# A rank matmul, a routing step and a tile layout moved in a three-stage kernel (long convolution, two expert layers) on one Trainium2 core

## The chip, the core and the metric

The kernel runs on one core of one Trainium2 chip. The metric is the device time of one execution in microseconds (us). The core has five engines that run their own instruction streams and meet at semaphores: TensorE (PE in the profile; PEld is its weight load), VectorE (DVE), ScalarE (ACT), GpSimd (POOL) and SyncE (SP), which issues most of the DMAs.

## What is computed

```python
# x, v: (2, 11456, 128); N = 2*11456 = 22912 tokens, D = 128, E = 8 experts, F = 1024
u = x * v;  h_filt = (relu(pos_emb @ w1) @ w2) * exp(-0.01 * pos)
y = causal_convolution(u, h_filt)      # by FFT over the sequence, per channel
x = (x * y).reshape(N, D)
# first expert layer: top-1 of 8
logits = x @ w_gate + modality_bias[modality_id];  e = argmax(logits)
out[t] = softmax(logits)[e] * (relu(x[t] @ w1[e]) @ w2[e])
# second expert layer: the same, routed by cosine similarity to expert_emb over tau
```

## The kernel before, in words

The program has four blocks, one after the other: `attention` (the convolution as small Fourier transforms on TensorE), `first_routing`, `experts` for the first layer (names `moe_...`, `router` true) and `experts` for the second (`moe2_...`). The change touches `first_routing`, `plan_tiles` by its place only, and the TensorE stream of `experts`.

**first_routing** works on `NB` = 184 blocks of 128 rows. TensorE transposes each block (line 951) and multiplies it with the gate weights (line 964), one DMA of 8 blocks at a time (`NU` = 23). The blocks are cut into the groups of `GROUPS`. When all logits of a group are there, VectorE runs `choose(j)` (line 1082 first, one-hot at line 1101), `gates(j)` (line 1108, after ScalarE's exponentials) and `places(j)` (lines 1122 to 1138, after TensorE's two rank matmuls, lines 974 and 975). `due(u)` says after which load TensorE and ScalarE serve a group: three loads after its last block, and never later than the end of the logits. After the last group VectorE works out the place of every row and splits it in a high and a low part, `hi` and `lo`.

Then the **matching loop**, `NM` = 23 rounds of `MG` = 8 blocks. In each, VectorE makes three bfloat16 tiles by comparing and multiplying (`at_lo` line 1188, `at_hi` line 1190, `lo_first` line 1193), ScalarE makes `lo_row` from `at_lo` (line 1036), and TensorE adds 16 matmuls of 208 columns into one bank (lines 992 and 994). The tiles lie in rings of `RING` = 3. Their innermost dimension has `LANES` = 2 blocks interleaved, so that TensorE reads one block with a stride of `LANES` elements. Ahead of the fourth round VectorE runs `plan_tiles`, some 25 small operations (first line 764, last line 808) that work out which tile of 512 rows belongs to which expert; the engines of `experts` read it as loop bounds. The loop ends with a cast of the bank into `k_where` (line 1196).

**experts** runs a loop over tiles of 512 tokens, 47 in the first layer. Per tile TensorE does `up(c)` for c = 0 to 7 (three matmuls each: hidden block c in two-term precision, into `ph`), `down(c)` (three each, accumulated in `po`), `send_back` of the previous tile (line 1440), and in the router layer `send_rank` (lines 697 and 699), which ranks the tokens of the previous tile within their next expert. `down` runs three blocks behind `up`; the third matmul of a `down` waits for VectorE's low part `h_lo` of that block (line 1639; the trace names it with line 1416). ScalarE makes the high part (`h_hi`, line 1518), copies `po` to `oT` (line 1567) when the last down block is done, and then copies `moe_o` to `moe_out` (line 1541, `copy_out`). VectorE fits the router's small operations between its `h_lo`: `factor` (from line 1662, after GpSimd's `moe_norm`, line 1780), `logits`, `best` (one-hot at line 682) and, at the tile's end, `place`. GpSimd takes the root for the norm, gathers the rows of a later tile (line 1761, four DMAs) and, once `moe_out` and the places are there, scatters the previous tile's rows (line 1751, four DMAs). Each engine takes its instructions in the order in which they are written: a wait holds up all that stands behind it.

`send_rank` waits for the one-hot of VectorE and for `moe_o`:

```python
def send_rank(g):
    if router:
        pe.wait_ge(oh_done, g + 1)
        pe.wait_ge(o_done, g + 2)
        r.rank(nc, k, prank).then_inc(rank_done, 1)
```

Of the kernel before, what the change touches and what calls it, by code (L numbers as in the profile page):

```python
# [52 lines left out]
TMAX = (N + NE * (T - 1)) // T  # L53
NHI = TA * (TMAX + 2)
NWG = 104
LANES = 2
ROUND = 1.5 * 2.0 ** 23


# [12 lines left out]
def host_tables():  # L72

    def rows(a, n):
# [27 lines left out]
        "before": f32(np.triu(np.ones((128, 128)), 1)), "not_after": f32(-np.tril(np.ones((128, 128)))),  # L102
        "count": f32(np.tile(np.repeat(np.arange(TA * TMAX), LANES), (128, 1))), "row": f32(np.arange(128) + 1)[:, None],
        "block": f32(128.0 * np.tile(np.arange(NB), (128, 1))), "descend": f32(NE - e), "regions": f32(CAP * e), "origin": f32(CAP * e - (BIG - 1)),
# [715 lines left out]
def first_routing(nc, io, k, att):  # L820
# [3 lines left out]
    XB = 6  # L824
    PB = 3
    GB = 48
    GROUPS = [(0, 48), (48, 48), (96, 48), (144, 32), (176, 8)]
    LATE = 3
    MG = 8
    RING = 3  # L830
    assert NU * UG == NB and sum(n for _, n in GROUPS) == NB
    table = att[1:1 + NB * 128].rearrange("(b p) d -> p b d", p=128)
    with ExitStack() as ctx:
        def sb(name, shape, dt=F32):
            return ctx.enter_context(nc.sbuf_tensor(f"r1_{name}", shape, dt))
# [4 lines left out]
        def sem(name):  # L840
            return ctx.enter_context(nc.semaphore(f"r1_{name}"))
# [24 lines left out]
        oh = sb("oh", [128, NE, NB], BF16)  # L866
        going = {n: sb(f"going{n}", [128, NE, n]) for n in sorted({n for _, n in GROUPS})}
        run = [sb(f"run{j}", [128, NE, n]) for j, (_, n) in enumerate(GROUPS)]
        place = sb("place", [128, NE, GB])
# [6 lines left out]
        lo = sb("lo", [128, NB], BF16)  # L876
        count_f = sb("count_f", [128, TA * TMAX * LANES])
        count = sb("count", [128, TA * TMAX, LANES], BF16)
        row = sb("row", [128, 1])
        first_f = sb("first_f", [128, NB])  # L880
        first = sb("first", [128, NB], BF16)
        at_hi = [sb(f"at_hi{n}", [128, MG // LANES, TA * TMAX, LANES], BF16) for n in range(RING)]
        at_lo = [sb(f"at_lo{n}", [128, MG // LANES, 128, LANES], BF16) for n in range(RING)]
        lo_first = [sb(f"lo_first{n}", [128, MG // LANES, 128, LANES], BF16) for n in range(RING)]
        lo_row = [sb(f"lo_row{n}", [128, MG // LANES, 128, LANES], BF16) for n in range(RING)]
# [27 lines left out]
        counted = sem("counted")  # L913
        planned = sem("planned")
# [3 lines left out]
        def due(u):  # L918

            return [j for j, (b, n) in enumerate(GROUPS) if min((b + n) // UG + LATE, NU + 1) == u]  # L920

# [3 lines left out]
        def _(sp):  # L925
# [8 lines left out]
            sp.dma_start(att[0:1, :], pad[:]).then_inc(meta_out, 16)  # L934
            for j, (b, n) in enumerate(GROUPS):
                sp.wait_ge(gate_done, j + 1)
                sp.dma_start(table[:, b:b + n, D:PITCH], meta[:, b:b + n, :]).then_inc(meta_out, 16)
            sp.wait_ge(meta_out, 16 * (len(GROUPS) + 1))

# [99 lines left out]
        def _(dve):  # L1039
            ch = Chain(dve, chain)  # L1040
# [118 lines left out]
            for e in range(1, NE):  # L1159
# [9 lines left out]
            ch.step(nc.vector.scalar_tensor_tensor(out=lo[:], in0=hi[:], scalar=-128.0, in1=pos[:],  # L1169
                                                   op0=ALU.mult, op1=ALU.add))  # L1170
            ch.settle()
            def lanes(x, m, n):

                return x[:, m * MG:(m + 1) * MG].rearrange("p (c a) -> p c a", a=LANES).unsqueeze(2).to_broadcast(
                    [128, MG // LANES, n, LANES])

            def counts(n):

                return count[:, 0:n, :].unsqueeze(1).to_broadcast([128, MG // LANES, n, LANES])

            for m in range(NM):
                q = m % RING
                if m == RING:
                    plan_tiles(nc, ch, k, counted, planned)
                if m >= RING:
                    dve.wait_ge(matched, m - RING + 1)
                    dve.wait_ge(lo_row_done, m - RING + 1)
                nc.vector.tensor_tensor(out=at_lo[q][:], in0=counts(128), in1=lanes(lo, m, 128), op=ALU.is_equal
                                        ).then_inc(lo_done, 1)
                nc.vector.tensor_tensor(out=at_hi[q][:], in0=counts(TA * TMAX), in1=lanes(hi, m, TA * TMAX),  # L1190
                                        op=ALU.is_equal)
                dve.wait_ge(lo_done, m + 1)
                nc.vector.tensor_tensor(out=lo_first[q][:], in0=at_lo[q][:], in1=lanes(first, m, 128), op=ALU.mult
                                        ).then_inc(hi_done, 1)
# [12 lines left out]
def experts(nc, io, k, name, src, router, dst):  # L1207
# [13 lines left out]
    with ExitStack() as ctx:  # L1221
# [6 lines left out]
        def sem(n):  # L1228
            return ctx.enter_context(nc.semaphore(f"{name}_{n}"))
# [77 lines left out]
        counted = sem("counted")  # L1307
        planned = sem("planned")
# [18 lines left out]
        def total(eng):  # L1327
            return eng.value_load(k.plan[0:1, ENDS + NE:ENDS + NE + 1], min_val=1, max_val=MAXT)
# [65 lines left out]
        @block.tensor  # L1394
        def _(pe):
            pe.sem_inc(xt_done, 1)
            pe.sem_inc(dn_done, HC)
            if router:
                pe.wait_ge(emb_unit, 1)
                nc.tensor.transpose(pback[:, 0, 0:128], emb[:], k.identity[:]).then_inc(emb_turned, 1)  # L1400
                pe.wait_ge(emb_ready, 1)

            def turn(n):

                pe.wait_ge(x_in, n * XN)
                for a in range(TA):
                    mm = nc.tensor.transpose(px[:, a * 128:(a + 1) * 128], x[:, a, 0:D], k.identity[:])  # L1407
                mm.then_inc(xt_done, 1)

            def passes(o, hi, lo, m_hi, m_lo, start, stop, rest):  # L1410

                nc.tensor.matmul(o, hi, m_hi, start=start, stop=False)  # L1412
                nc.tensor.matmul(o, lo, m_hi, start=False, stop=False)  # L1413
                if rest:
                    pe.wait_ge(*rest)
                return nc.tensor.matmul(o, hi, m_lo, start=False, stop=stop)  # L1416

            def up(g, q, c):

                pe.wait_ge(hlo_done, g * HC + (HC + c - 3))  # L1420
                w = slice(c * 128, (c + 1) * 128)
                passes(ph[c % 4][:], w_hi[q][:, 0, w], w_lo[q][:, 0, w], x_hi[:], x_lo[:], True, True,
                       (xlo_done, g + 1) if c == 0 else None).then_inc(up_done, 1)

            def down(g, q, c):
                pe.wait_ge(hhi_done, g * HC + (c + 1))
                w = slice(c * 128, (c + 1) * 128)
                passes(po[:], w_hi[q][:, 1, w], w_lo[q][:, 1, w], h_hi[c][:], h_lo[c][:], c == 0, c == HC - 1,
                       (hlo_done, g * HC + (HC + c + 1))).then_inc(dn_done, 1)

            def send_back(g):

                pe.wait_ge(ot_done, g + 1)
                pe.wait_ge(o_done, g + 1)
                if router:
                    pe.wait_ge(placed, g + 1)
                for a in range(TA):
                    to, cols = pgroups[:, a // 2, a % 2, :], oT[:, a * 128:(a + 1) * 128]
                    if router:
                        mm = nc.tensor.matmul(to, cols, to_rows[:], start=True, stop=True)  # L1440
                    else:
                        mm = nc.tensor.transpose(to, cols, k.identity[:])  # L1442
                mm.then_inc(back_done, 1)
# [7 lines that stand above are left out]
            turn(1)  # L1451

            def body(g, q, s, start):
                pe.wait_ge(w_ready, s * 2 + 1 if router else start * 2 + 1)
                pe.wait_ge(xhi_done, g + 1)
                for c in range(3):
                    up(g, q, c)
                send_back(g)
                pe.wait_ge(w_ready, s * 2 + 2 if router else start * 2 + 2)
                for c in range(3, HC):  # L1460
                    if c == (3 if router else HC - 1):
                        turn(g + 2)
                    up(g, q, c)
                    down(g, q, c - 3)
                down(g, q, HC - 3)
                down(g, q, HC - 2)
                send_rank(g)
                down(g, q, HC - 1)

            sections(pe, None, body)  # L1470
            g = total(pe)
            send_back(g)
            send_rank(g)
# [389 lines left out]
```

## Time and profile before

| | |
|---|---|
| runs | 2071.11, 2071.28, 2074.29 us (median 2071.28) |
| profiled execution | 2071.28 us, of which the span of its instructions 2069.5 us |
| mean granted TensorE clock | 0.961 |
| busy share of the span | TensorE 91%, VectorE 72%, ScalarE 56%, GpSimd 44% |

All times in the rows are microseconds from the start of the span, unless marked ns. A row of the timeline gives start, duration, engine, line, operation, what it writes and reads, shapes, a count where several like ones are merged, and in brackets how long the engine had been idle before it and what released it. The ends of matmuls are modelled, so that one seems to run into the next; the distance of their starts says how fast they come. Matmuls of line 1412, 1413 and 1416 are the first, second and third of an `up` (into `moe_ph`) or a `down` (into `moe_po`).

### The profile page before, as it was taken

The numbers are of one execution on the slowest core, as the hardware profiler recorded it, in microseconds if no ns is written. First come the engines' busy times: TensorE is split into PE (matmuls) and PEld (weight loads), VectorE is DVE, ScalarE is ACT, GpSimd is POOL, SyncE is SP. The second block draws the span as 40 slices with busy tenths as digits, with TensorE's granted clock in tenths as the row PEclk, the third lists the DMA queues.
The fourth block names the chain that finished last, engine by engine and source line by source line (L and its number), as shares of the span: only waits on it lengthen the run. The fifth ranks groups of instructions, "written<-read, shape, count | busy, mean of one in ns | idle before, by whom it ended". The sixth has DMA issues, their size and how long they took to land. (4 is left out here: it accounts for less than half of the span.)

```text
span 2069.5 us, 37272 instructions
## 1 busy us (share of the span) xinstructions
PE 1875.3 (91%) x10049; PEld 1457.8 (70%) x10050; DVE 1482.8 (72%) x3249; ACT 1165.5 (56%) x2462; POOL 909.0 (44%) x879
## 2 busy tenths in 40 slices
PE   8999999999848659999999999984799999999996
PEld 5777777767538547777777777763687787888785
DVE  4759999999925946666666666664677777777775
ACT  1885555555413436666666666553566666666664
POOL 1455555555210036666666666654333232333333
PEclk9999999999969879999999999997899999999998
DMA  2003555555478011111111111124212112111121
GB/s 85 1 24 89 122 123 123 123 123 124 81 168 171 4 61 35 44 44 41 44 44 44 41 45 42 42 59 62 72 46 63 57 46 94 41 46 45 42 64 47
DMA packets 233640, 138.06 MB, mean 67 GB/s; under 512 B 142442, under 2 KB 221364, under 8 KB 233444
## 3 DMA queue, kind: packets, MB, share of 16 engines
q1 hardware_dynamic: 207506, 95.45, 19.9%
q0 software_dynamic: 22080, 39.76, 7.0%
q10 hardware_dynamic: 3986, 2.00, 0.5%
q8 instruction: 37, 0.61, 0.1%
q14 instruction: 31, 0.25, 0.0%
HBM read 96.17 MB, written 43.36 MB: 67 GB/s over the span
## 5 line engine op out<-in xcount | busy, mean ns | idle before, releaser
L1639 DVE SCALAR_TENSOR_TENSOR moe_h_lo<-moe_ph,moe_h_hi 128x512 fp32r<-128x512 f32 x760 | 506.7, 687 | 285.6 <-ACT moe_h_hi L1518 216.2
L1518 ACT ACTIVATE moe_h_hi<-moe_ph 128x512 fp32r<-128x512 f32 x760 | 444.7, 602 | 211.4 <-PE moe_ph L1416 169.9
L1751 POOL DMA_INDIRECT out<-moe_o,moe_idx x200 | 196.9, 984 | 425.5 <-DVE moe_o L1654 361.9
L1412 PE MATMUL moe_ph<-moe_x_hi,moe_w_hi 128*128 128x512 f32 x760 | 320.5, 422 | 18.9 <-issue 16.8
L1416 PE MATMUL moe_po<-moe_h_lo,moe_w_hi 128*128 128x512 f32 x760 | 307.7, 405 | 22.0 <-DVE moe_h_lo L1639 14.6
L1412 PE MATMUL moe_po<-moe_h_hi,moe_w_hi 128*128 128x512 f32 x760 | 304.6, 401 | 0.0
L1416 PE MATMUL moe_ph<-moe_x_lo,moe_w_hi 128*128 128x512 f32 x760 | 302.7, 398 | 0.0
L1413 PE MATMUL moe_ph<-moe_x_hi,moe_w_lo 128*128 128x512 f32 x760 | 301.6, 397 | 0.0
L1413 PE MATMUL moe_po<-moe_h_hi,moe_w_lo 128*128 128x512 f32 x760 | 298.6, 393 | 0.0
L1761 POOL DMA_INDIRECT moe_x<-attention,moe_at x196 | 201.0, 1025 | 208.5 <-issue 195.2
L1751 POOL DMA_INDIRECT rows<-moe_out,moe_r_idx x196 | 195.5, 997 | 181.0 <-ACT moe_out L1541 125.7
L1416 PEld LDWEIGHTS moe_po<-moe_h_lo,moe_w_hi 128*128 128x128 f32 x760 | 143.0, 188 | 87.3 <-DVE moe_h_lo L1639 36.1
L1412 PEld LDWEIGHTS moe_ph<-moe_x_hi,moe_w_hi 128*128 128x128 f32 x760 | 145.0, 191 | 59.5 <-issue 35.6
L320 PEld LDWEIGHTS ps<-dft_rows_sb,W 107*119 107x119 f32 x1536 | 172.4, 186 | 19.9 <-issue 19.9
L320 PE MATMUL ps<-dft_rows_sb,W 107*119 107x108 f32 x1536 | 177.7, 270 | 6.7 <-DVE W L450 5.5
L1416 PEld LDWEIGHTS moe_ph<-moe_x_lo,moe_w_hi 128*128 128x128 f32 x760 | 144.6, 190 | 34.6 <-DVE moe_x_lo L1625 0.2
L1413 PEld LDWEIGHTS moe_po<-moe_h_hi,moe_w_lo 128*128 128x128 f32 x760 | 143.2, 188 | 31.4
L1567 ACT ACTIVATE moe_oT<-moe_po 128x512 f32<-128x512 f32 x95 | 56.8, 598 | 192.1 <-PE moe_po L1416 192.1
L1413 PEld LDWEIGHTS moe_ph<-moe_x_hi,moe_w_lo 128*128 128x128 f32 x760 | 145.3, 191 | 25.2
L1412 PEld LDWEIGHTS moe_po<-moe_h_hi,moe_w_hi 128*128 128x128 f32 x760 | 143.2, 188 | 28.1 <-ACT moe_h_hi L1518 0.3
L333 PE MATMUL ps<-A,dft_cols_sb 119*109 119x432 f32 x384 | 155.3, 526 | 0.3 <-DVE POOLED L482 0.3
L590 POOL TENSOR_TENSOR U<-X,V 107x440 f32<-107x440 f32 x64 | 71.8, 1122 | 176.7 <-DVE POOLED L527 174.3
(210 smaller groups left out, 3165.5 us busy)
## 6 DMA issues: line engine op xcount, KB each, us to landing
moe_x<-rows SPq DMA_DIRECT2D x49, 260.0 KB
X<-in_x SPq DMA_DIRECT2D x64, 192.5 KB, 5.3
V<-in_v SPq DMA_DIRECT2D x64, 192.5 KB, 4.2
XF<-in_xf SPq DMA_DIRECT2D x64, 192.5 KB, 2.6
moe_w_raw<-in_moe_w SPq DMA_DIRECT2D x24, 512.0 KB
r_x<-attention SPq DMA_DIRECT2D x23, 512.0 KB, 6.8
attention<-POOLED SPq DMA_DIRECT2D x48, 220.0 KB
out<-moe_o,moe_idx POOLq DMA_INDIRECT x200
```

Of the source, the lines that this page charges most:

```text
L320: mm = nc.tensor.matmul(p[0:KW, a, c * 2 * H1:(c + 1) * 2 * H1], W[g % 2][0:N1, a, c, 0:KW], dft_rows[0:N1, :], start=True, stop=True)
L333: mm = nc.tensor.matmul(p[0:N2, x, 0:F4], dft_cols[0:KW, x * N2:(x + 1) * N2], A[g % 2][0:KW, :, :, x, :].rearrange("p a c f -> p (a c) f" ...
L590: nc.gpsimd.tensor_tensor(out=U[t % 2][:, 0], in0=X[t % NX][0:N1], in1=V[t % NX][0:N1], op=ALU.mult).then_inc(u_ready, 1)
L1412: nc.tensor.matmul(o, hi, m_hi, start=start, stop=False)
L1413: nc.tensor.matmul(o, lo, m_hi, start=False, stop=False)
L1416: return nc.tensor.matmul(o, hi, m_lo, start=False, stop=stop)
L1518: nc.scalar.activation(h_hi[c][:], ph[c % 4][:], ACT.Relu).then_inc(hhi_done, 1)
L1567: nc.scalar.activation(oT[:], po[:], ACT.Copy).then_inc(ot_done, 1)
L1639: nc.vector.scalar_tensor_tensor(out=h_lo[c][:], in0=ph[c % 4][:], scalar=0.0, in1=h_hi[c][:].bitcast(F32), op0=ALU.max, op1=ALU.subtract) ...
L1751: pool.indirect_dma_start(dst, bass.IndirectOffsetOnAxis(ap=idx[:, a:a + 1].bitcast(U32), axis=0), out[:, a, 0:width], None, bounds_check= ...
L1761: pool.indirect_dma_start(x[:, a, :], None, src, bass.IndirectOffsetOnAxis(ap=at[:, a:a + 1].bitcast(U32), axis=0), bounds_check=NB * 128, ...
```

## The change

Four edits. `LANES` goes from 2 to 4: the tiles of the matching loop interleave four blocks instead of two, and the table `count` (and the input it is cast from) doubles. `GROUPS` has a last group of 40 blocks in place of one of 32 and one of 8. `plan_tiles` is called ahead of the matching loop instead of ahead of its fourth round. In `experts`, `send_rank(g)` is called ahead of the last three down blocks instead of ahead of the last one.

```diff
-LANES = 2
+LANES = 4
...
-    GROUPS = [(0, 48), (48, 48), (96, 48), (144, 32), (176, 8)]
+    GROUPS = [(0, 48), (48, 48), (96, 48), (144, 40)]
...
             ch.settle()
+            plan_tiles(nc, ch, k, counted, planned)
+
             def lanes(x, m, n):
...
             for m in range(NM):
                 q = m % RING
-                if m == RING:
-                    plan_tiles(nc, ch, k, counted, planned)
                 if m >= RING:
...
                     up(g, q, c)
                     down(g, q, c - 3)
+                send_rank(g)
                 down(g, q, HC - 3)
                 down(g, q, HC - 2)
-                send_rank(g)
                 down(g, q, HC - 1)
```

## Rows read from the trace of the kernel before

**Rows 1.** The page, busy us (share of the span) and instructions, TensorE
```profile
PE 1875.3 (91%) x10049; PEld 1457.8 (70%) x10050; DVE 1482.8 (72%) x3249; ACT 1165.5 (56%) x2462; POOL 909.0 (44%) x879
```

**Rows 2.** Windows: busy us and count by engine, clock, DMA share, GB/s
```profile
664.23:679.64 15.41, 0.68 (x4) 0.24 (x4) 13.96 (x51) 0.67 (x2) 0.00 (x0) 0.66 0.47 72
679.64:735.10 55.46, 41.02 (x368) 35.22 (x368) 53.30 (x92) 26.44 (x23) 0.00 (x0) 0.91 0.00 1
```

**Rows 3.** Timeline of the groups, first operation of each and the last logits
```profile
619.33 0.56 DVE L1082 TENSOR_TENSOR r_lg<-r_psl,r_bias 128x384 f32<-128x384 f32 x1 [5.08 <-PE r_psl L964]
...
660.50 3.72 PE L964 MATMUL r_psl<-r_wg,r_xT 128*128 128x104 f32 x32
...
664.23 0.42 DVE L1082 TENSOR_TENSOR r_lg<-r_psl,r_bias 128x256 f32<-128x256 f32 x1
...
670.57 0.22 DVE L1082 TENSOR_TENSOR r_lg<-r_psl,r_bias 128x64 f32<-128x64 f32 x1
...
674.17 0.16 DVE L1148 TENSOR_SCALAR r_room<-r_run 128x8 f32<-128x8 f32 x1
```

**Rows 4.** Timeline of VectorE: plan_tiles and the start of two rounds
```profile
686.06 0.15 DVE L764 TENSOR_TENSOR k_nth<-k_cursor,k_origin 1x8 f32<-1x8 f32 x1
...
690.08 0.69 DVE L1188 TENSOR_TENSOR r_at_lo<-r_count,r_lo 128x1024 bf16<-128x1024 bf16 x1
...
692.23 0.68 DVE L1188 TENSOR_TENSOR r_at_lo<-r_count,r_lo 128x1024 bf16<-128x1024 bf16 x1
```

**Rows 5.** Matching loop, groups by form (busy us, mean ns, idle before); two matmuls
```profile
L1190 DVE TENSOR_TENSOR r_at_hi<-r_count,r_hi 128x1664 bf16<-128x1664 bf16 x23 | 23.4, 1018 | 0.0
L994 PEld LDWEIGHTS r_psx<-r_at_hi,r_lo_row 128*128 128x128 bf16 x184 | 19.0, 103 | 0.6
...
L1188 DVE TENSOR_TENSOR r_at_lo<-r_count,r_lo 128x1024 bf16<-128x1024 bf16 x23 | 15.8, 685 | 0.0
...
724.85 0.25 PE L992 MATMUL r_psx<-r_at_hi,r_lo_first 128*128 128x208 bf16 x1
...
724.94 0.25 PE L994 MATMUL r_psx<-r_at_hi,r_lo_row 128*128 128x208 bf16 x1
```

**Rows 6.** Timeline, router layer: one h_lo, TensorE's down blocks 5 and 7, the rank
```profile
1009.10 0.68 DVE L1639 SCALAR_TENSOR_TENSOR moe_h_lo<-moe_ph,moe_h_hi 128x512 fp32r<-128x512 f32 x1
...
1009.84 0.50 PE L1416 MATMUL moe_po<-moe_h_lo,moe_w_hi 128*128 128x512 f32 x1 [0.18 <-DVE moe_h_lo L1639]
...
1011.52 0.19 PE L697 MATMUL moe_pback<-moe_r_oh,k_before 128*128 128x40 bf16 x1
...
1011.66 0.48 PE L1412 MATMUL moe_po<-moe_h_hi,moe_w_hi 128*128 128x512 f32 x1
...
1011.97 0.40 PE L1413 MATMUL moe_po<-moe_h_hi,moe_w_lo 128*128 128x512 f32 x1
...
1012.21 0.40 PE L1416 MATMUL moe_po<-moe_h_lo,moe_w_hi 128*128 128x512 f32 x1
```

**Rows 7.** The same tile and the next one-hot, other engines
```profile
1007.18 0.17 DVE L1662 TENSOR_SCALAR moe_scale<-moe_norm 128x4 f32<-128x4 f32 x1 [1.60 <-POOL moe_norm L1780]
...
1010.33 0.19 DVE L682 TENSOR_TENSOR moe_r_oh<-k_descend,moe_r_km 128x32 bf16<-128x32 f32 x1
...
1011.36 1.01 POOL L1761 DMA_INDIRECT moe_x<-attention,moe_at  x1 [0.30 <-issue]
...
1013.13 0.63 ACT L1541 ACTIVATE moe_out<-moe_o 128x520 f32<-128x520 f32 x1
...
1023.75 0.19 DVE L682 TENSOR_TENSOR moe_r_oh<-k_descend,moe_r_km 128x32 bf16<-128x32 f32 x1
```

**Rows 8.** Timeline of ScalarE at the end of the next tile
```profile
1026.61 0.60 ACT L1567 ACTIVATE moe_oT<-moe_po 128x512 f32<-128x512 f32 x1 [2.75 <-PE moe_po L1416]
1027.10 0.64 ACT L1541 ACTIVATE moe_out<-moe_o 128x520 f32<-128x520 f32 x1
```

**Rows 9.** Groups of ScalarE, 780 to 1360 us; idle before in us
```profile
L1567 ACT ACTIVATE moe_oT<-moe_po 128x512 f32<-128x512 f32 x42 | 25.1, 598 | 104.6 <-PE moe_po L1416 104.6
```

## The prediction

> **What bounds the kernel now.** I read the page first [rows 1]: TensorE is busy 91% of the span, so most of the kernel is TensorE work that this change leaves alone. Its granted clock dips in one place, between the attention and the first expert layer, and three of the four edits are there. So I took windows by stage [rows 2]: from 664.23 to 679.64 us, where the routing numbers are made, TensorE works 0.68 us and VectorE 13.96 of 15.41; from 679.64 to 735.10, the matching loop, VectorE works 53.30 of 55.46 us and TensorE 41.02. VectorE is the bound of both. The fourth edit is in the first expert layer, which I read tile by tile in the timeline [rows 6, 7].
>
> In such a tile TensorE's third matmul of down block 5 waits 0.18 us at 1009.84 for VectorE's h_lo. VectorE is late because it had waited 1.60 us for GpSimd's norm (row at 1007.18). GpSimd is late because it first issues four scatters of the tile before, and these wait for ScalarE's copy to moe_out. That copy waits for oT, and oT for TensorE's last down matmul. So there is a closed loop: one-hot (its end, called T here, is 1010.33 + 0.19 = 1010.52), last down matmul 1012.21, copy 1013.13, scatters, norm, one-hot again at T = 1023.94. That is 13.42 us a tile, and TensorE's small stalls are its slack. Whatever lies between T and the copy counts in full, once a tile.
>
> **The parts.**
>
> *Five groups become four, the last of 40.* Groups 0 to 2 keep their sizes. Now VectorE takes the group of 32 from 664.23 to 670.57, 6.34 us, and the group of 8 to 674.17, 3.60, together 9.94 [rows 3]. Both are the same chain of small operations, so the cost per block is (6.34 - 3.60) / 24 = 0.114 us, and 40 blocks take 6.34 + 8 x 0.114 = 7.25. What is lost is a head start: the new group needs the very last logits, whose matmuls end at 660.50 + 3.72 = 664.22. VectorE comes free at 664.23 anyway, so with a handover it starts at 664.3. Gain 9.94 - 7.25 - 0.09 = **2.6 us**; the ends are 2.2 (a later handover, or one return from another engine that is late) and 2.8.
>
> *plan_tiles ahead of the loop.* It is 4.0 us of VectorE (686.06 to 690.08) wherever it stands [rows 4]. VectorE runs the 23 rounds of 2.15 us (690.08 to 692.23) almost without a wait, so the sum is the same. TensorE now starts 4 us later, with the same work per round, and the final matmuls follow VectorE's last round as before. **0**, from -0.2 (TensorE no longer pauses in mid-loop) to +0.5 (its first rounds, at the half clock, use up the ring of three).
>
> *LANES 2 to 4.* The same instructions over the same elements; only the order inside a tile changes, and the stride at which TensorE reads, from 4 to 8 bytes. VectorE takes 1018 ns for the 1664 elements of at_hi and 685 for the 1024 of at_lo [rows 5]: 640 more in 333 ns, 1.92 per ns. If a pair per step is its full rate, runs of four bring nothing; I expect no gain. TensorE's matmuls come 0.09 us apart (724.85, 724.94) and may take 2.15 / 16 = 0.134 before they set the pace. No row has an 8-byte stride. The lower end is 0.09, no cost. For the upper I take the widest reads in the trace: 512 contiguous four-byte columns every 0.235 us [rows 6] are 8.7 bytes of range per ns, and 208 columns at 4 bytes in 0.09 are 9.2. If range were the limit, 8 bytes would take 0.19, a round 3.04, and 21 rounds 21 x 0.89 = 19 us more. I take the lower end, because per column both rows are alike too (2.2 and 2.3 per ns), that is, skipping every second element has cost nothing so far. The weight loads (103 ns) lie beside the matmuls. The table of counts doubles, 0.2 MB more; its load and cast lie in VectorE's idle time before 619.33, 5.08 us [rows 3]. **0**.
>
> The Trainium skill, page "SBUF — State Buffer", section "Door 1: The DMA port swizzle", says that SBUF is read in lines of 16 bytes and that the full rate needs at least two hits in a line. Eight bytes are just at that limit: by the rule the edit costs 0 and the sum stands, by the upper bound it would be 19 us more. No row here shows it.
>
> *The rank moved ahead of two down blocks.* It takes its wait for the one-hot along, and what stands behind it in TensorE's queue, down blocks 5, 6 and 7 and then the next tile, waits too. Down 4 is issued by about 1009, one-hot comes at 1010.52: TensorE stands still for 1.5 us (about 1.0 once the period has grown). Before, it did blocks 5 and 6 in that time. New timing from T, by the gaps of [rows 6]: start of the rank +0.06 (h_lo ends 1009.78, its matmul starts 1009.84), first down matmul +0.14, second +0.31, third +0.24, six more at 0.235 = 1.41. The last starts at T + 2.16, where it was T + 1.69. So **+0.47 us on the loop** for a tile like this.
>
> But there are two kinds of tile. In this one the copy starts at 1013.13, T + 2.61. In the next [rows 8] it starts at 1027.10, T + 3.16, with the down matmuls no later after T: their release comes late. ScalarE's mean idle before oT over 42 tiles is 104.6 / 42 = 2.49 us [rows 9]; between 2.20 for the prompt kind (1012.64 less the end of its x_hi copy at 1010.44) and about 2.75 for the late one, that makes some 20 prompt tiles and 22 late. oT starts there at 1026.61, T + 2.67. GpSimd's fourth gather starts 1011.36, T + 0.84 in every tile I looked at, so I read the late release as tied to GpSimd's work, about 1.8 us after that gather began, and not to the matmul. Then the late tiles lose nothing: the new last matmul ends at 2.16 + 0.40 = T + 2.56, still before it. They may gain up to 0.1. Sum: 21 prompt tiles (one more near the end of the layer) x 0.47 = 9.9, less 22 x 0.05 = 1.1 for the late, **+8.8 us**. Ends: 7.7, and 43 x 0.47 = 20.2 if the lateness adds to the matmul.
>
> *Sum.* 2071.28 (the profiled run's own time, which is also the median of the three; its span is 2069.5) - 2.6 + 0 + 0 + 8.8 = **2077.5**.
>
> **Rivals.** *The lateness adds to the matmul:* I don't see what holds the release back, and if it is something of TensorE's own it will still come after the last matmul. Against it: its time fits GpSimd's. 2071.3 - 2.6 + 20.2 = 2088.9.
>
> *The moved rank costs nothing.* A TensorE that pauses may post its releases at once in every tile, and this would pay the 9.9 back: 22 late tiles x 0.55 = 12.1, less the 1.1 already counted, offsets most or all of it. Or the pace of the layer is held elsewhere. 2071.3 - 2.6 = 2068.7.
>
> *TensorE becomes the bound of the matching loop,* by the 8-byte stride and above 0.134 us a matmul. 2077.5 + 19 = 2096.5. For it: no row reads so wide a range; against: columns, not range, have set the pace so far.
>
> *Faster:* the rank's increment, queued ahead of down 7's, is what holds the release; moved away it clears all 22 late tiles, 12.1 us, and the wait is hidden as well. It decides only if the one-hot is there when down 4 ends, 1.5 us earlier after the norm than the rows show. 2071.3 - 2.6 - 12.1 = 2056.6.
>
> **How the numbers follow.** The forecast has 0.50, with a range of its own of 2075 to 2081; lateness adds 0.17; the rank costs nothing 0.13; stride 0.10; faster 0.08; the last 0.02 is what I can't name. A measurement of this kernel can tell about 0.2% from no change, 4.1 us. Slower by more: 0.50 + 0.17 + 0.10 = 0.77; within: 0.13 + 0.02 = 0.15; faster: 0.08. The range leaves out the stride and the faster case: 2068 to 2090, holding 0.80.
>
> **What would show it.** In the new profile the rank's first matmul, line 697, waits for VectorE's one-hot in nearly every tile, about 1 us each; every copy to moe_out starts T + 3.05 to 3.2, and the period is 13.9 us in all tiles; VectorE does the last group from 664.3 to about 671.6; a round of the loop stays 2.14 to 2.15 us with matmuls 0.09 apart, and VectorE's last round ends 2.6 us earlier. What would make it wrong: copies at T + 3.6 (lateness adds), rounds near 3 us (stride), no wait ahead of line 697, or copies at T + 2.6 in all tiles.

## The result, and the profile after

| | before | after |
|---|---|---|
| median (lowest to highest), us | 2072.78 (2071.11 to 2074.86), 4 runs | 2103.27 (2100.5 to 2107.57), 4 runs |
| ratio, 95% interval | | 1.0148 (1.0128 to 1.0170) |
| profiled execution, its span | 2071.28, 2069.5 | 2087.48, 2085.7 |

Slower by 1.5%, 30.5 us, where the forecast was 2077.5 and the range ended at 2090. The profiled execution of the changed kernel lies 16 us below its timed runs. The runs below came on three chips, here A (the first four kernels), B (the next four) and C (the last four), on which the kernel before took 2045.52 (15 runs), 2075.59 (15) and 2048.17 (29). What differs between them is in the first expert layer and behind it, and the profile of the changed kernel looks there like chips A and C, that of before like chip B. So this profile is compared with that of before ahead of that layer, and from there on with care.

The page of the changed kernel, the line of busy times, beside [rows 1]:

```profile
PE 1883.0 (90%) x10047; PEld 1469.6 (70%) x10048; DVE 1480.7 (71%) x3231; ACT 1169.9 (56%) x2461; POOL 908.9 (44%) x879
```

Almost nothing is to be seen there, since it is an average over stages. The same two stages as in [rows 2], as windows of the changed kernel (columns as there), show it:

```profile
665.23:681.96 16.73, 0.45 (x2) 0.11 (x2) 15.32 (x56) 0.47 (x1) 0.00 (x0) 0.62 0.43 66
681.96:753.52 71.56, 69.23 (x368) 43.25 (x368) 50.91 (x71) 26.44 (x23) 0.00 (x0) 0.95 0.00 1
```

The matching loop holds fewer VectorE instructions than before, 71 for 92, since plan_tiles has left it, and yet takes 71.56 us where it took 55.46. TensorE works 69.23 us of it for 41.02, with the same 368 matmuls: the bound has changed engines. The timeline of VectorE from the last group to the first round answers to [rows 3, 4]:

```profile
665.23 0.49 DVE L1082 TENSOR_TENSOR r_lg<-r_psl,r_bias 128x320 f32<-128x320 f32 x1
...
672.48 0.16 DVE L1148 TENSOR_SCALAR r_room<-r_run 128x8 f32<-128x8 f32 x1
...
677.94 0.15 DVE L764 TENSOR_TENSOR k_nth<-k_cursor,k_origin 1x8 f32<-1x8 f32 x1
...
681.96 0.68 DVE L1188 TENSOR_TENSOR r_at_lo<-r_count,r_lo 128x1024 bf16<-128x1024 bf16 x1
```

The last group takes 672.48 - 665.23 = 7.25 us, where two took 9.94; plan_tiles takes its 4.02 us ahead of the loop.

A table of all stages, each worked out from the first rows of its two ends in the timeline of VectorE: the last groups (line 1082 to line 1148), from there to the first round (line 1188), the loop (to the cast at line 1196), the router layer (first to last one-hot, line 682) and what follows it, to the end of the span. The last three kernels come in the section on the experiments.

| span of, us | last groups | to the loop | loop | router layer | after it |
|---|---|---|---|---|---|
| before | 9.94 | 5.47 | 55.08 | 656.77 | 638.5 |
| after | 7.25 | 9.48 | 71.55 | 662.36 | 630.9 |
| after again, chip B | 7.26 | 9.49 | 71.56 | 669.21 | 637.7 |
| LANES alone, chip A | 9.92 | 5.47 | 73.07 | 639.81 | 630.3 |
| rank alone, chip C | 9.93 | 5.47 | 55.08 | 663.84 | 629.7 |

The last two columns are where the chips differ. All others repeat to 0.02 us from one execution to the next, so a stage of VectorE's and TensorE's own work can be read from one trace.

### The profile page after: what moved, and what is told of

It reads as the page before. It is cut to its first block and busy times, and to the rows that moved or that the text cites. A ratio compares the mean times of both kernels' runs of the same rounds, so it can differ in the third digit from the quotient of the medians.

```text
span 2085.7 us, 37243 instructions
## 1 busy us (share of the span) xinstructions
PE 1883.0 (90%) x10047; PEld 1469.6 (70%) x10048; DVE 1480.7 (71%) x3231; ACT 1169.9 (56%) x2461; POOL 908.9 (44%) x879
## 5 line engine op out<-in xcount | busy, mean ns | idle before, releaser
L1518 ACT ACTIVATE moe_h_hi<-moe_ph 128x512 fp32r<-128x512 f32 x760 | 449.8, 603 | 180.6 <-PE moe_ph L1416 171.2
L1412 PE MATMUL moe_ph<-moe_x_hi,moe_w_hi 128*128 128x512 f32 x760 | 315.3, 415 | 13.4 <-issue 11.4
L1416 PE MATMUL moe_po<-moe_h_lo,moe_w_hi 128*128 128x512 f32 x760 | 301.0, 396 | 4.3 <-DVE moe_h_lo L1639 4.3
```

The lines of the kernel that those rows point to most:

```text
L1518: nc.scalar.activation(h_hi[c][:], ph[c % 4][:], ACT.Relu).then_inc(hhi_done, 1)
```

## Experiments

### The changed kernel with LANES at 2, and each edit alone (chip A)

```diff
 # e1_lanes2: the changed kernel with
-LANES = 4
+LANES = 2
 # e2_rank_alone: the kernel before with
                     down(g, q, c - 3)
+                send_rank(g)
                 down(g, q, HC - 3)
                 down(g, q, HC - 2)
-                send_rank(g)
 # e3_lanes4_alone: the kernel before with
-LANES = 2
+LANES = 4
 # e4_groups_plan: the kernel before with
-    GROUPS = [..., (144, 32), (176, 8)]
+    GROUPS = [..., (144, 40)]
...
+            plan_tiles(nc, ch, k, counted, planned)
...
-                if m == RING:
-                    plan_tiles(nc, ch, k, counted, planned)
```

> The changed kernel with LANES back at 2, the other three edits kept. Theory 1 (the 8-byte stride makes TensorE the bound of the matching loop, 0.187 us a matmul): the loop takes 2.14 us a round again and about 20 us go away; the profiled execution comes to 2087.5 - 20 = 2067 or, with the rank's 7 us seen in the changed profile, about 2076 against a before of 2071. Rival (the loop is slow because plan_tiles now stands ahead of it and TensorE starts late and cold): the loop keeps rounds of 3.0 us and the time stays within 5 us of the changed kernel's. Open besides: the changed kernel's timed runs (median 2103.3) are 16 us above its profiled one (2087.5). If that belongs to the stride, this kernel's timed runs agree with its profiled one at 2076; if it belongs to the rank, they stand near 2092.

> The kernel before with the rank moved alone. Theory 1 (0.46 us more on the loop for prompt tiles, nothing for late ones): every copy to moe_out starts 3.07 us after the one-hot, period 13.86, and the time is 2079, 7 to 8 us above before. Rival (the lateness adds in executions other than the profiled one): timed 2090 to 2095, with the profiled one at 2079.

> The kernel before with LANES 4 alone. Theory 1: rounds of 3.0 us with TensorE without a pause, 19 to 20 us more, 2091. Rival (the stride matters only together with the late start): rounds of 2.14 us and 2071. The 16 us between timed and profiled runs of the changed kernel: if they belong to the stride they appear here, 2107 timed beside 2091 profiled.

> The kernel before with the four groups and plan_tiles ahead of the loop, LANES 2 and the rank where it was. Theory 1: 1.6 to 2.6 us less, 2069, the gain all in VectorE's last group, and the move of plan_tiles worth nothing within 0.5 us. Rival (the late, cold start of TensorE costs several us in the loop): 2073 or more, with VectorE waiting for TensorE in the first rounds.

| | median, us | to before on the chip, us | ratio (95%) |
|---|---|---|---|
| LANES 2 in the changed kernel | 2068.26 | +22.7 | 1.0112 (1.0096 to 1.0127) |
| rank alone | 2068.28 | +22.8 | 1.0114 (1.0099 to 1.0130) |
| LANES 4 alone | 2064.54 | +19.0 | 1.0092 (1.0076 to 1.0107) |
| groups and plan_tiles | 2044.53 | -1.0 | 0.9995 (0.9986 to 1.0004) |

Two edits cost, and they add up: 2045.5 + 22.8 + 19.0 - 1.0 = 2086.3, beside the 2087.5 of the profiled execution of the changed kernel. LANES is the edit that the forecast had at nothing. In the changed kernel, the matching loop goes like this, VectorE's and TensorE's timelines:

```profile
717.48 0.69 DVE L1188 TENSOR_TENSOR r_at_lo<-r_count,r_lo 128x1024 bf16<-128x1024 bf16 x1 [0.78 <-PE r_psx L994]
...
720.48 0.69 DVE L1188 TENSOR_TENSOR r_at_lo<-r_count,r_lo 128x1024 bf16<-128x1024 bf16 x1 [0.77 <-PE r_psx L994]
...
722.14 0.37 PE L992 MATMUL r_psx<-r_at_hi,r_lo_first 128*128 128x208 bf16 x1
...
722.33 0.37 PE L994 MATMUL r_psx<-r_at_hi,r_lo_row 128*128 128x208 bf16 x1
```

A matmul every 0.19 us, so 16 of them take 3.0 us, which is the distance of VectorE's rounds; and VectorE, which had waited for nothing in [rows 4], now waits 0.77 us a round for TensorE to free a ring slot. The groups by form of the same stretch answer to [rows 5]:

```profile
L992 PE MATMUL r_psx<-r_at_hi,r_lo_first 128*128 128x208 bf16 x184 | 67.7, 368 | 15.2 <-DVE r_lo_first L1193 15.2
...
L994 PEld LDWEIGHTS r_psx<-r_at_hi,r_lo_row 128*128 128x128 bf16 x184 | 21.6, 118 | 12.8
```

TensorE's idle time, 15.2 us, lies ahead of its first matmul but for 2.3 at most, since the window of the loop has it busy for 69.23 of 71.56 us. VectorE's instruction for at_hi has the same row as in [rows 5], 1018 ns: runs of four bring it nothing, as forecast. The weight load has grown from 103 to 118 ns, which is less than the 0.134 us that a matmul may take before TensorE sets the pace.

Alone in the kernel before, LANES 4 lengthens the loop by 73.07 - 55.08 = 18.0 us; in the changed kernel, against the same kernel with LANES 2 (whose loop is 51.05), by 20.5. The 2.5 between them is the move of plan_tiles. In the loop, TensorE, now the slower one, has work in hand for most of VectorE's 4 us, and the loop is only 73.07 - 71.55 = 1.5 us longer for them; ahead of the loop they are paid in full: 9.48 + 71.55 = 81.03 us from the end of the groups to the cast, beside 5.47 + 73.07 = 78.54. With LANES at 2 the move costs nothing (9.49 + 51.04 beside 5.47 + 55.08).

### Which operand, and is there a step (chip B)

The kernel before with LANES 8, then with the width of the moving operand (`at_hi`, the tile whose columns a matmul streams through) and of the weights (`at_lo`, `lo_first`, `lo_row`) set apart, LH and LL; and the changed kernel again, unaltered, since its profile and its times had come apart.

```diff
 # e6_lanes8
-LANES = 2
+LANES = 8
 # e7_hi4_lo2; e8_hi2_lo4 has 2, 4
+LH, LL = 4, 2
-        at_hi = [sb(f"at_hi{n}", [128, MG // LANES, TA * TMAX, LANES], BF16) for n in range(RING)]
-        at_lo = [sb(f"at_lo{n}", [128, MG // LANES, 128, LANES], BF16) for n in range(RING)]
+        at_hi = [sb(f"at_hi{n}", [128, MG // LH, TA * TMAX, LH], BF16) for n in range(RING)]
+        at_lo = [sb(f"at_lo{n}", [128, MG // LL, 128, LL], BF16) for n in range(RING)]
...
-                for c in range(MG // LANES):
-                    for a in range(LANES):
+                for b in range(MG):
+                    hi_b = at_hi[q][:, b // LH, :, b % LH]
```

> The changed kernel again, unaltered. Theory 1 (the two costs are 20 us for the stride and about 20 us for the rank where a chip shows no late releases, as it was in the four runs before this one, and 7 to 9 us where it does): if this chip's before stands near 2045, 2088; if it stands near 2072, 2100 to 2103. Rival (the parts are not additive: two costs together come to the 30 us first measured): 2076 beside 2045.

> The kernel before with LANES 8: TensorE reads with a stride of 16 bytes, one column in each 16-byte piece. Theory 1 (what counts is the range of bytes that a matmul passes over, about 8.9 per ns): a matmul every 0.37 us, rounds of 6.0, the loop 138 us, 80 us more than before. Rival (one step: 4 bytes are free, and any wider stride halves the rate): 0.187 us, as with LANES 4, and 18 us more.

> Only the moving operand at_hi interleaves four blocks (8 bytes); the weights lo_first and lo_row keep two. Theory 1 (the moving read is what is slow): 0.187 us a matmul, rounds of 3.0, 18 us more than before. Rival (it is the weight load): 0.093 us, rounds of 2.14, no change.

> The reverse: weights at 8 bytes, moving operand at 4. Theory 1: 0.093 us a matmul, rounds of 2.14, no change; the weight load, 103 ns at 4 bytes and 118 at 8, lies beside the matmuls. Rival (weight load): 0.187 us and 18 us more.

| | median, us | ratio (95%) | loop, us | between matmuls, us |
|---|---|---|---|---|
| changed kernel again | 2103.07 | 1.0132 (1.0110 to 1.0154) | 71.56 | 0.19 |
| LANES 8 | 2158.84 | 1.0407 (1.0380 to 1.0435) | 139.91 | 0.37 |
| moving operand 4 wide | 2091.00 | 1.0069 (1.0042 to 1.0096) | 72.86 | 0.19 |
| weights 4 wide | 2074.83 | 0.9993 (0.9981 to 1.0004) | 55.12 | 0.09 |

TensorE's timeline with LANES 8:

```profile
740.03 0.56 PE L994 MATMUL r_psx<-r_at_hi,r_lo_row 128*128 128x208 bf16 x1
740.41 0.55 PE L992 MATMUL r_psx<-r_at_hi,r_lo_first 128*128 128x208 bf16 x1
740.78 0.55 PE L994 MATMUL r_psx<-r_at_hi,r_lo_row 128*128 128x208 bf16 x1
```

The same with only the moving operand 4 wide:

```profile
724.89 0.37 PE L993 MATMUL r_psx<-r_at_hi,r_lo_first 128*128 128x208 bf16 x1
...
725.08 0.37 PE L995 MATMUL r_psx<-r_at_hi,r_lo_row 128*128 128x208 bf16 x1
```

And with only the weights 4 wide, its timeline, and then its group by form:

```profile
724.89 0.25 PE L993 MATMUL r_psx<-r_at_hi,r_lo_first 128*128 128x208 bf16 x1
...
724.98 0.25 PE L995 MATMUL r_psx<-r_at_hi,r_lo_row 128*128 128x208 bf16 x1
```
```profile
L995 PEld LDWEIGHTS r_psx<-r_at_hi,r_lo_row 128*128 128x128 bf16 x184 | 21.7, 118 | 0.4
```

The moving operand does it alone. At a stride of 4, 8 and 16 bytes a matmul of 208 columns comes every 0.093, 0.187 and 0.373 us: 208 x 4 / 0.093, 208 x 8 / 0.187 and 208 x 16 / 0.373 are each 8.9 bytes of range per ns. So at 8 and 16 bytes it is the range of memory swept that counts, and not the columns; at 4 bytes and the full clock the two would give the same pace, and no run tells them apart there. With the weights at 8 bytes the load takes 118 ns for 103 and costs nothing on the end. It takes 118 to 119 as well where only the moving operand is 4 wide, so the load time is not a matter of the weights' stride alone.

The granted clock has to be ruled out as the cause, for it isn't the same in all three. In these windows the first pair behind the bounds is TensorE's busy time and matmuls, and the third number from the end is its granted clock. Windows of the changed kernel (8 bytes) early and late in the loop, and then of LANES 8:

```profile
684.00:688.00 4.00, 3.76 (x21) 2.56 (x22) 4.00 (x7) 2.19 (x2) 0.00 (x0) 0.50 0.00 0
...
704.00:708.00 4.00, 4.00 (x23) 2.52 (x22) 2.92 (x5) 1.50 (x2) 0.00 (x0) 1.00 0.01 2
```
```profile
740.00:750.00 10.00, 10.00 (x28) 3.93 (x27) 3.59 (x5) 2.15 (x2) 0.00 (x0) 0.50 0.00 1
```

At 8 bytes the clock stands at 0.50 in the first rounds and at 1.00 later, and the matmuls come 0.187 us apart in both: the pace doesn't follow the clock. At 4 bytes it does, 0.173 at the half clock in the first rounds of the kernel before and 0.093 at the full one. With LANES 8 the clock stays at 0.50 through the whole loop, although TensorE shows no idle time. Since columns at that clock need only 0.173 us, the 0.373 is again the stride's; that it would be so at the full clock too, no run shows.

The Trainium skill, page "SBUF — State Buffer", section "Door 1: The DMA port swizzle", has the full rate for two hits in a line of 16 bytes. The runs differ: two hits a line (8 bytes) give half the pace of four, one hit (at a granted clock of 0.50) a quarter. The measurement decides.

### Where the rank may stand (chip C)

The kernel before with the rank one down block earlier (ahead of down 6, between the old place and the new one), then one down block later (behind the last), the latter with the group of 40 as well, and once more where the change puts it.

```diff
 # e9_rank_mid          # the lines from the loop over c on
                 down(g, q, HC - 3)
+                send_rank(g)
                 down(g, q, HC - 2)
-                send_rank(g)
                 down(g, q, HC - 1)
 # e10_rank_last (and e11_groups_rank_last, with (144, 40) in GROUPS)
-                send_rank(g)
                 down(g, q, HC - 1)
+                send_rank(g)
 # e12_rank_alone_again: as e2_rank_alone
```

> The kernel before with the rank one down block earlier (ahead of block 6) instead of two. Theory 1 (what counts is how long after the one-hot's end T the last down matmul starts): TensorE reaches the rank about when the one-hot is there, then three gaps of the first block and three of 0.235 follow, so the last down matmul starts at T + 1.46 instead of T + 1.69; the period falls from 13.41 by 0.23 and the time by 43 x 0.23 = 10 us where releases are prompt, less where they are late. Rival (any earlier place of the rank costs, because a wait is put ahead of down matmuls): slower than before, by a few us.

> The kernel before with the rank behind the last down block. Theory 1: the last down matmul starts at T + 1.37, and the time falls by up to 43 x 0.32 = 14 us, unless TensorE's own 13.0 us of work per tile becomes the bound first. Rival (VectorE needs the rank for the places and now waits for it, so that the scatter waits for the places instead of for the copy): no gain or a loss, with a wait of VectorE ahead of its place operation.

> The rank behind the last down block and the four groups (32 and 8 joined), all else as before. Theory 1: the two gains add, 2 to 3 us below the kernel with the rank last alone. Rival: they don't show beside the scatter of the runs.

> The rank moved alone, as in the second run, once more. Theory 1 (the cost depends on the chip: 20 to 23 us where before stands near 2045, 10 to 13 us where it stands near 2072, because late tiles lose little): the ratio follows the level of before on this chip. Rival (the cost is one and the same, and the first measured pair hid something else): 22 us whatever before is.

| rank | median, us | ratio (95%) | median period, us |
|---|---|---|---|
| ahead of down 5 (the change) | 2070.61 | 1.0117 (1.0103 to 1.0132) | 13.87 |
| ahead of down 6 | 2048.83 | 1.0001 (0.9993 to 1.0010) | 13.43 |
| ahead of down 7 (before, from LANES alone) | 2048.17 | | 13.41 |
| behind down 7 | 2048.11 | 1.0000 (0.9991 to 1.0008) | 13.42 |
| behind down 7, group of 40 | 2044.90 | 0.9990 (0.9981 to 0.9999) | 13.43 |

I had expected 10 us less with the rank ahead of down 6, and up to 14 less with it behind down 7; neither came. Behind the last down block, the copy to moe_out does start earlier, but the loop doesn't get shorter. The timeline of that kernel, a tile whose one-hot ends at T = 1004.47:

```profile
1006.89 0.64 ACT L1541 ACTIVATE moe_out<-moe_o 128x520 f32<-128x520 f32 x1
...
1007.52 0.16 DVE L713 SCALAR_TENSOR_TENSOR moe_r_idx<-moe_meta_b,moe_r_pos 128x4 int32<-128x4 f32 x1
...
1008.56 1.02 POOL L1751 DMA_INDIRECT rows<-moe_out,moe_r_idx  x1 [2.26 <-DVE moe_r_idx L713]
```

The copy starts at T + 2.42 and no longer at T + 2.61, yet the scatter stays at T + 4.09, since VectorE's places (the row of line 713) end at T + 3.21. The waits of GpSimd's scatters over the layer have changed their cause, first in the kernel before, then in this one (what it waited for, us in total, times, longest):

```profile
POOL rows L1751 <- ACT moe_out L1541: 109.9, 42, 5.7
```
```profile
POOL rows L1751 <- DVE moe_r_idx L713: 95.0, 42, 2.3
```

With the rank one down block earlier the copy starts at T + 2.43 too and the period is the same, though in the trace two of the tiles after a change of the expert (told below) take 14.3 to 14.4 us; timed, it is level with the kernel before.

So the loop has a second branch, from the one-hot over VectorE's places to the scatters. In the tile of [rows 7] the copy ends at T + 3.24, and the places, in nearly every tile, at T + 3.21 to 3.22: the two are some 0.03 us apart. A later copy counts in full, an earlier one gives nothing.

The group of 40 with the rank last is the only version whose interval lies below 1, and only just: it is 3.3 us of 2048 below the kernel before. Its loop and its layer are those of the kernel before, and its groups take 7.25 us, so that the 2.7 us of the groups account for most of it. The same groups on chip A, with plan_tiles moved, were timed 1.0 us below, with an interval that holds no change.

## Why the prediction was wrong, point by point

**Groups, right.** Forecast 9.94 to 7.25 less a handover of 0.09; all five traces with four groups have 7.25 or 7.26, and in the changed kernel VectorE starts within 0.03 us of the last logits. The 2.7 us are read from the traces of that stage; the timed runs alone hardly resolve them.

**plan_tiles at 0, right only while VectorE is the bound.** With LANES at 2 it is 0; with LANES at 4 it costs 2.5 us of the loop. The forecast gave the edits one by one and did not ask what the cover is once another engine sets the pace.

**LANES at 0, wrong, and the step that failed.** The prediction had the right bounds, 0 and 19, and a threshold, 0.134 us a matmul, with which all runs agree. The failed step is the choice between them: "I take the lower end, because per column both rows are alike too". The two rows, 512 columns of 4 bytes and 208 bfloat16 columns at a stride of 4 bytes, were alike in columns per ns *and* in range per ns (8.7 and 9.2). They have the same stride in bytes, so they could not tell the two apart, and "skipping every second element has cost nothing so far" says nothing of a wider skip. Measured: 0.187 a matmul where range as the limit gave 0.19, a round of 3.00 where it gave 3.04, and 18.0 to 20.5 us where it gave 19. The rival with chance 0.10 had this mechanism and its price; its 2096.5 for the kernel falls short of 2103.3 by what the rank and plan_tiles cost beyond the forecast and by the 1.5 us more that the kernel before took in the comparison.

**Rank, the mechanism right, the size off by its rare tiles.** The timeline of a tile in the changed kernel answers to [rows 6, 7]; T is 1005.02 + 0.19 = 1005.21:

```profile
1005.27 0.19 PE L697 MATMUL moe_pback<-moe_r_oh,k_before 128*128 128x40 bf16 x1 [0.91 <-DVE moe_r_oh L682]
...
1007.35 0.39 PE L1416 MATMUL moe_po<-moe_h_lo,moe_w_hi 128*128 128x512 f32 x1
1007.78 0.60 ACT L1567 ACTIVATE moe_oT<-moe_po 128x512 f32<-128x512 f32 x1 [2.65 <-PE moe_po L1416]
1008.26 0.16 DVE L713 SCALAR_TENSOR_TENSOR moe_r_idx<-moe_meta_b,moe_r_pos 128x4 int32<-128x4 f32 x1
1008.28 0.63 ACT L1541 ACTIVATE moe_out<-moe_o 128x520 f32<-128x520 f32 x1
```

The wait ahead of line 697 is there, 0.91 us (forecast about 1.0); the last down matmul starts at T + 2.14 (forecast 2.16), the copy at T + 3.07 (3.05 to 3.2), and the period is 13.87 (13.9). The waits of TensorE between 780 and 1360 us of the changed kernel show it in nearly all of the tiles (us in total, times, longest):

```profile
PE moe_pback L697 <- DVE moe_r_oh L682: 37.6, 40, 1.4
```

The two kinds of tile are real too. One-hots in the timeline of the kernel before:

```profile
955.45 0.19 DVE L682 TENSOR_TENSOR moe_r_oh<-k_descend,moe_r_km 128x32 bf16<-128x32 f32 x1
...
968.87 0.20 DVE L682 TENSOR_TENSOR moe_r_oh<-k_descend,moe_r_km 128x32 bf16<-128x32 f32 x1
...
982.90 0.19 DVE L682 TENSOR_TENSOR moe_r_oh<-k_descend,moe_r_km 128x32 bf16<-128x32 f32 x1
...
996.31 0.19 DVE L682 TENSOR_TENSOR moe_r_oh<-k_descend,moe_r_km 128x32 bf16<-128x32 f32 x1
```

They come 13.42, 14.03 and 13.41 us apart: prompt and late tiles take turns. Set against the changed kernel on chip B, period by period, the 42 periods in the body of the layer give: 17 prompt ones +8.76 us (0.52 each, forecast 0.47), 22 late ones -1.24 (-0.06 each, forecast -0.05), and 3 that the forecast did not have apart, +6.07. The five at the ends give -1.16; sum 12.4, beside a forecast of 8.8. The rank alone was not run on chip B, but the three kernels there that leave it in its place have 656.6 to 657.4 us for this layer, and the changed one 669.2.

The three are those that follow a change of the expert, in which TensorE stands still twice. The timeline of TensorE in the changed kernel, and then the windows up to the end of its second stop and behind it (the granted clock is again the third number from the end):

```profile
974.13 0.50 PE L1416 MATMUL moe_po<-moe_h_lo,moe_w_hi 128*128 128x512 f32 x1 [1.18 <-DVE moe_h_lo L1639]
...
976.02 0.19 PE L697 MATMUL moe_pback<-moe_r_oh,k_before 128*128 128x40 bf16 x1 [1.39 <-DVE moe_r_oh L682]
...
977.29 0.63 PE L1412 MATMUL moe_po<-moe_h_hi,moe_w_hi 128*128 128x512 f32 x1
977.72 0.63 PE L1413 MATMUL moe_po<-moe_h_hi,moe_w_lo 128*128 128x512 f32 x1
```
```profile
970.00:976.40 6.40, 3.83 (x20) 2.63 (x19) 3.41 (x13) 2.14 (x5) 5.28 (x6) 1.00 0.15 46
976.40:979.90 3.50, 3.50 (x10) 2.69 (x10) 2.94 (x13) 0.00 (x0) 1.08 (x2) 0.51 0.19 47
```

After stops of 1.18 and 1.39 us the granted clock falls to 0.51, that is to 1.2 GHz, the down matmuls come 0.43 us apart instead of the 0.235 of [rows 6], and the copy of this tile starts 4.6 us after the one-hot. The next period is 15.40 us. It doesn't fall at every change: in the changed kernel's own profile the third such period is 13.87, and on chip B the second is 13.84. With the rank alone the third is 13.87 on chip A, and on chip C all three are hit (15.17, 15.39, 15.31; together +5.65 over those of LANES alone). The stops are as long where the clock holds, as the third such tile of the changed kernel shows:

```profile
1370.75 0.19 PE L697 MATMUL moe_pback<-moe_r_oh,k_before 128*128 128x40 bf16 x1 [1.39 <-DVE moe_r_oh L682]
```
```profile
1371.00:1374.50 3.50, 3.50 (x18) 2.82 (x17) 3.07 (x13) 1.23 (x3) 1.24 (x2) 1.00 0.61 52
```

Here the earlier stop was 1.19 us. So what makes the clock fall at one change and not at another stays open. I had priced the wait by what it does in a tile with the clock at 1.00. The step that was mis-sized is "21 prompt tiles x 0.47 less 22 x 0.05": it holds for the tiles it names, but in these three, for which it has 1.4 us, the traces show 3.9 to 6.1.

On chips A and C there are no late tiles: with LANES alone all periods of the body but those at an expert's end are 13.40 to 13.44. There the rank has 42 prompt tiles to lengthen, and costs 22.4 to 22.8 us: set against LANES alone, the trace of chip C has 39 x 0.455 = 17.7, 5.65 for the three, and 0.7 at the ends, in all 24.0, that of chip A 22.4. That is near the 20.2 that the prediction had for a wait counted in every tile, though its reason there (lateness that adds) is not what happens.

**The sum.** On chip B 2075.6 - 2.7 + 20.5 + 12.4 = 2105.8, beside the 2103.1 and 2103.3 that the changed kernel took. Of the 25.8 us between forecast and result, 20.5 are LANES with plan_tiles, 3.6 the rank, and 1.5 that the kernel before measured 2072.8 in the comparison and not 2071.3.

**The rivals.** That the rank costs nothing is refuted on all chips. That the lateness adds to the matmul is refuted too: with the last down matmul at T + 2.14 the copies of chip B would start near T + 3.6, and in nearly all tiles they start at T + 3.05 to 3.20, about where the late ones of the kernel before start with that matmul at T + 1.69. That the rank gains by clearing the late releases is not borne out: where releases are late, the late tiles stay at 13.9. What holds a release back stays open. It is there or not by the chip, with the same program. With the rank in its old place the mean wait ahead of oT is 105.3 / 42 = 2.51 us on chip B (weights 4 wide) and 92.1 / 42 = 2.19 on chip A (LANES alone). The groups of line 1567, which is 1568 in the kernel of chip B, chip B first:

```profile
L1568 ACT ACTIVATE moe_oT<-moe_po 128x512 f32<-128x512 f32 x42 | 25.1, 599 | 105.3 <-PE moe_po L1417 105.3
```
```profile
L1567 ACT ACTIVATE moe_oT<-moe_po 128x512 f32<-128x512 f32 x42 | 25.1, 599 | 92.1 <-PE moe_po L1416 92.1
```

My reading of it as tied to GpSimd's gathers was only argued from the times within a tile; no run here moved the gathers, so it was not tried.

## What to carry to other kernels

Where two rows agree on a rate, ask whether they differ in the quantity that the edit changes; if both have the same value of it, they leave the choice open, and then the upper bound deserves a large share of the chance, not a tenth. A cover is a property of the whole kernel: an edit that costs nothing beside the bound of today may be charged in full once another edit has moved the bound. And in a loop over several engines look for the second-longest branch before pricing a move: here it lay some 0.03 us behind the first, so that a copy some 0.46 us later in every tile cost 18 of the 22 us and one 0.19 us earlier gave nothing.

## What the runs showed of the hardware that was not expected

- The pace of matmuls goes with the stride of the moving operand: 0.093, 0.187 and 0.373 us for 208 bfloat16 columns at 4, 8 and 16 bytes, and at 8 bytes it is 0.187 at either level of the clock. With either operand at 8 bytes the weights load in 118 ns instead of 103; weights at 8 bytes change nothing else.
- The same program takes 2045 to 2048 us on two chips and 2076 on a third. In the traces compared here, the layer with GpSimd's indirect DMAs carries it: 640 or 657 us in the router layer, 630 or 638 behind it; the matching loop before it repeats to 0.02 us.
- With LANES 8 the granted clock stayed at 0.50 through 140 us in which TensorE went from one matmul to the next without a gap. With LANES 4 it rose to 1.00 in the first rounds.
- Stops of TensorE of 1.18 and 1.39 us within one tile were followed by 3.5 us at a granted clock of 0.51; after stops of 1.19 and 1.39 us two experts later, in the same execution, it stayed at 1.00.
